# First expert layer in six units of two chunks and four of three, with seven short items to an attention slot, on one Trainium2 core

## What is computed

```python
for t in range(S):                      # 768 steps, 4 x 8 heads of 48
    S_re, S_im = ar*S_re - ai*S_im + k[t] (x) v[t],  ar*S_im + ai*S_re
    y[t] = q[t] @ S_re                  # a = (ar, ai), its magnitude clipped at 0.999
x = y as 3072 tokens x 384
h = x @ w_in                            # 384 -> 2048
x = (h * clip(h + 3, 0, 6) / 6) @ w_out # first layer
h = x @ w2_in
out = (max(h, 0) + alpha * min(h, 0)) @ w2_out   # second layer
```

## Time and profile before

| what | value |
|---|---|
| median of 3 runs | 1022.65 us (1019.16 to 1023.57) |
| the profiled execution's own time | 1022.65 us |
| its span, first to last instruction | 1020.9 us |
| busy: PE, PEld | 964.2 us, 864.4 us |
| busy: DVE, ACT, POOL | 598.6, 481.7, 265.5 us |
| mean granted TensorE clock | 0.986 of full speed |

### The profile page before, as it was taken

How to read it: one execution, slowest core, us unless ns; L and a number is a source line. 1 busy time by engine, 2 the same in 40 slices (tenths; PEclk the granted TensorE clock), 3 DMA queues, 4 the chain that set the end, 5 groups by cost and what they waited for, 6 DMA issues and landing times.

```text
span 1020.9 us, 17091 instructions
## 1 busy us (share of the span) xinstructions
PE 964.2 (94%) x6498; PEld 864.4 (85%) x6498; DVE 598.6 (59%) x1088; ACT 481.7 (47%) x865; POOL 265.5 (26%) x235
## 2 busy tenths in 40 slices
PE   0789988999999999999999999999999999999997
PEld 0678888889999999999999998888888888888886
DVE  6858888788787878878772245443433433434332
ACT  7746777666677667677742453221221222212211
POOL 0000122222222222322222333333333333323332
PEclk9789999999999999999999999999999999999999
DMA  6762323334333333432321701000010010100000
GB/s 168 204 148 71 87 71 83 94 86 118 76 94 84 76 94 96 97 94 71 82 68 24 272 31 55 0 31 33 1 63 1 1 62 1 62 1 1 32 1 31
DMA packets 80931, 70.49 MB, mean 69 GB/s; under 512 B 32592, under 2 KB 78160, under 8 KB 80464
## 3 DMA queue, kind: packets, MB, share of 16 engines
q1 hardware_dynamic: 77648, 66.42, 23.9%
q10 hardware_dynamic: 3200, 2.97, 1.2%
HBM read 40.90 MB, written 9.44 MB: 49 GB/s over the span
## 4 chain that ended last, share of the span: by engine, by line
PE 74%; DVE 10%; SPq 5%; ACT 4%; issue 3%; DMA 2%; DVEq 0%; ACTq 0%
PE op L1202 11%; PE op L1203 10%; PE hp L1203 10%; PE op L1204 10%; PE hp L1202 10%; PE hp L1204 10%; PE yp L1190 3%; SPq L413 2%; PE gp L1197 2%; DMA st<-prod 2%; PE op L1250 2%; PE gp L1169 2%; DVE t_fb L820 2%; SPq L416 1%; PE hp L1225 1%
## 5 line engine op out<-in xcount | busy, mean ns | idle before, releaser
L535 POOL TENSOR_TENSOR g_lo<-gated,g_hi 128x384 fp32r<-128x384 f32 (+2 forms) x224 | 263.3, 1176 | 746.0 <-ACT g_hi L631 746.0
L631 ACT ACTIVATE g_hi<-gated 128x384 fp32r<-128x384 f32 (+2 forms) x224 | 123.0, 549 | 327.2 <-DVE gated L918 284.4
L914 DVE TENSOR_SCALAR gate<-hp,alpha_sb 128x512 f32<-128x512 f32 x96 | 72.1, 751 | 239.9 <-PE hp L1204 239.9
L903 DVE SCALAR_TENSOR_TENSOR gated<-gate,hp 128x384 f32<-128x384 f32 (+1 forms) x144 | 72.9, 506 | 130.8 <-ACT gate L624 130.7
L1202 PE MATMUL op<-g_hi,wb_hi 128*128 128x384 f32 (+1 forms) x384 | 129.4, 337 | 2.9 <-POOL g_lo L535 2.6
L1202 PE MATMUL hp<-x_hi,wa_hi 128*128 128x384 f32 (+1 forms) x384 | 127.1, 331 | 3.8 <-DVE gated L903 2.9
L1204 PE MATMUL op<-g_hi,wb_lo 128*128 128x384 f32 (+1 forms) x384 | 124.5, 324 | 0.0
L1203 PE MATMUL op<-g_lo,wb_hi 128*128 128x384 f32 (+1 forms) x384 | 124.3, 324 | 0.0
L1203 PE MATMUL hp<-x_lo,wa_hi 128*128 128x384 f32 (+1 forms) x384 | 123.8, 322 | 0.0
L1204 PE MATMUL hp<-x_hi,wa_lo 128*128 128x384 f32 (+1 forms) x384 | 123.8, 322 | 0.0
L624 ACT ACTIVATE gate<-hp,half 128x384 f32<-128x384 f32 (+1 forms) x144 | 76.8, 533 | 95.7 <-PE hp L1204 81.0
(11 more groups left out here) (110 smaller groups left out, 1652.1 us busy)
## 6 DMA issues: line engine op xcount, KB each, us to landing
st<-prod SPq DMA_DIRECT2D x76, 145.1 KB, 3.0
a_sb<-a_in SPq DMA_DIRECT2D x24, 288.0 KB, 3.9
qk_sb<-qk_in SPq DMA_DIRECT2D x24, 288.0 KB, 3.6
v_pad<-v_in SPq DMA_DIRECT2D x24, 192.0 KB, 4.1
x_raw<-x SPq DMA_DIRECT2D x6, 768.0 KB, 5.6
out<-out_sb SPq DMA_DIRECT2D x6, 768.0 KB, 4.0
st<-prod SPq DMA_DIRECT2D x96, 32.2 KB, 2.3
wa_raw<-w_in SPq DMA_DIRECT2D x6, 512.0 KB, 6.4
```

The lines of the kernel that those rows point to most:

```text
L535: pool.tensor_tensor(g_lo[:, at, 0:wide], gated[:, at * UT:at * UT + wide], g_hi[:, at, 0:wide].bitcast(F32), ALU.subtract).then_inc(glo_d ...
L631: act.activation(g_hi[:, at, 0:wide], gated[:, at * UT:at * UT + wide], ACT.Copy).then_inc(ghi_done, 1)
L903: dve.scalar_tensor_tensor(out=gated[:, to], in0=gate[:, at], scalar=1.0, in1=hp[:, n % 2, 0:wide], op0=ALU.min, op1=ALU.mult).then_inc(ga ...
L914: dve.tensor_scalar(gate[:, at], hp[:, n % 2, 0:wide], 0.0, alpha_sb[:, m:m + 1], ALU.min, ALU.mult).then_inc(gate_done, 1)
```

## The change

The first layer has ten units in place of nine: six of two chunks and four of three, where three of two and six of three stood. It has 160 items in place of 144. Three items in place of two come ahead of the first slot, whose length goes from 7 to 6. Slots 3 to 10 have 7 items, slots 11 to 14 have 8, 7, 7 and 8, all of units of two chunks; before, slots 3 and 4 had 7, slots 5 to 8 had 6 (two-chunk units) and slots 9 to 14 had 5, 5, 6, 5, 5, 6 (three-chunk units). In long slots `forward` of a chunk moves from the end of the slot before to the first item of its own, and `squares` moves one item later (letter "s").

```diff
-SIZES = (2, 2, 2, 3, 3, 3, 3, 3, 3)
+SIZES = 6 * (2,) + 4 * (3,)
...
-SHORT = {6: ("a", "cf", "deo", "glv", "hij", "kb"), 7: ("a", "cf", "deo", "glv", "hi", "j", "kb")}
-LONG = {5: ("a", "cdefg", "ov", "hij", "klb"), 6: ("a", "cdefg", "ov", "hij", "klb", "")}
...
-ALONE = 2
-LENGTHS = (7, 7, 7, 6, 6, 6, 6) + 4 * (5, 5, 6) + (5, 6, 6)
+SHORT = {6: ("a", "cf", "deos", "glv", "hij", "kb"), 7: ("a", "cf", "deos", "glv", "hi", "j", "kb"),
+         8: ("a", "cf", "deos", "glv", "hi", "j", "kb", "")}
+LONG = {5: ("aB", "cdefg", "ov", "hijs", "kl"), 6: ("aB", "cdefg", "ov", "hijs", "kl", "")}
...
+ALONE = 3
+LENGTHS = (6,) + 8 * (7,) + (8, 7, 7, 8) + 2 * (5, 5, 6) + (5, 6, 6)
...
+            if s > FIRST and is_short(s - 1):
+                steps = steps.replace("B", "")
...
-                if "o" in steps and c3 is not None:
+                if "s" in steps and c3 is not None:
                     squares(c3)
...
-            gate1(3)
+            for n in range(1, ALONE):
+                gate1(n + GSTEP)
...
                     fractions(c1)
+                    if "B" in steps:
+                        forward(c1)
```

## The result

The changed kernel took 1019.13 us (median of 20 runs, 1014.28 to 1023.22) against 1022.68 us (20 runs) for the kernel before: a ratio of 0.9966, 95% interval [0.9953, 0.9979]. It is faster by 3.5 us where 9.6 were forecast, and 0.13 us above the range. The profiled execution took 1018.77 us, span 1017.1 us.

The account below looks back on a forecast made before the run. PE was taken as nearly always busy after the first third, with losses to win before slot 15. Terms -4.3 (start of slot 3), -0.8 (slots 4 to 8), -4.5 (slots 9 to 14) took 1022.65 to 1013.0 us; range 1008.5 to 1019.0.

Parts of the forecast that it names:

- the term 21.5 us for slot 6: Slot 6 with seven items for six: PE needs 20.6 us, 21.5 taken, a little over the need.
- the store of unit 1: On SP ahead of slot 6's restack: one item earlier than before, so it lets go sooner; no separate size given.
- The attention chain holds the short slots: Rival, slots 6 to 14: engines set the length, 22.6 us per seven-item slot; 1024.2 us, half of it 1018.6; chance 0.15.
- slots 9 to 14: Six slots now of two-chunk items: 130.6 us together against 135.1 before, a term of -4.5 us.
- slot 4: Seven items and seven weight splits in both orders: keeps its 23.56 us.
- slot 5: A seventh item fits into the 2.38 us wait at its end; DVE limits it, 25.3 us.
- slot 8: Seven items for six: PE needs 21.2 us, 21.5 taken.
- the price of a two-chunk item: PE's time per item of a two-chunk unit: 2.16 us, against 3.12 us for a three-chunk one.
- Items of one price at any width: Rival: weight loads bound PE, so 16 more items cost 3.12 us each; 1059.1 us, chance 0.01.
- the step with DVE and ACT in all short slots: Slower rival: seven-item slots run at slot 4's 23.56 us; 1031.6 us, chance 0.05.
- three items ahead: Before slot 2: extra item cuts PE's wait from 3.88 to 1.3 us, restores the clock; slot 3 starts 4.3 us earlier.
- letters "B" and "s": Moved `forward` and `squares` in long slots: taken at nothing; rival of a loss at unit borders, 1017.0 us, chance 0.04.

Follow-up runs that it names:

- leave_first: Changed kernel with ACT's copy of unit 1's sums moved ahead of the other steps of its item; 1013.43 us, ratio 0.9932.
- third_item: Changed kernel with slot 5 at six items and slot 6 at eight, so unit 1 ends in slot 6's third item; 1016.04 us, ratio 0.9945.
- old_letters: Changed kernel with `forward` and `squares` of the long slots back where they stood before; 1020.57 us, ratio 0.9987.
- dose_three: leave_first with three table loads (3.84 us of ACT work) ahead of the early copy of unit 1's sums; 1018.48 us, ratio 0.9977.
- alone_three: Kernel before with only three items ahead of slot 2 and six in it; 1019.44 us, ratio 0.9985.

## Why the prediction was wrong

- **The step that failed: slots 6 to 8, the term 21.5 us for slot 6.** Measured were 27.96, and 23.07 with the copy early. The prediction looked at what stands beside slot 6 on SP ("the store of unit 1 ... behind the second item now and not the third, so it lets go sooner") and missed that the same move puts ACT's copy behind `logs`, 3.4 us behind its gate, with `output(32)` waiting for it on PE. leave_first and third_item, two edits that share only this, take PE's wait away. leave_first comes to 1013.43 us where 1013.0 had been forecast; part of that nearness is luck, since its own kernel before was faster as well, and it gained 8.3 of the 9.6 us.
- **What it cost, in the profile.** PE's need in slot 6 is 20.6; 0.68 and 2.39 of waits make 23.7; the other 4.3 us are the low clock, 10.2 us long (with 3.4 us of it, in old_letters, 1.8). Against leave_first slot 6 is 4.9 us longer and slot 7 22.49 - 21.14 = 1.35. That is 6.2 us in these two executions, where the medians give 4.8 to 5.7 and the ratios 3.5: the changed kernel's profile has the longest low clock seen behind this wait.
- **The other half of slot 6's term** was small: without the late copy it took 23.07, because the chain and not PE ends it. "The attention chain holds the short slots" was right for this one and wrong for slots 8 to 14, in which PE is busy for over 99% of the time.
- **Right: slots 9 to 14** (130.79 for 130.6), slot 4 (23.56 for 23.56), slot 5 (25.14 for 25.3), slot 8 (21.13 for 21.5), the price of a two-chunk item (slot 9 with seven of them took 21.39 us, with PEld busy for 20.76 of it). Items of one price at any width are out; so is the step with DVE and ACT in all short slots.
- **Right in its place and off in its size: three items ahead.** The wait fell from 3.88 to 0.64 us, further than to 1.3, and the clock in slot 2 is 1.00. Slot 3 begins 5.9 us earlier where 4.3 were taken; of the 1.1 us kept back for DVE, 0.7 show one slot later (slot 3 took 24.65 us where 23.93 were taken). In medians it is 2.3 to 2.8: the sum took the wait of 3.88 us from one profile, and other executions of the same order have 2.34 and 0.65. So this term of the sum was 1.5 to 2 us too large for a median, next to the late copy the second part of the miss.
- **Off: letters "B" and "s".** Taken at nothing, they gain 1.0 us in the changed kernel; half of it makes good what the rest of the change adds there, and slot 15 to the end took 656.1 us where 656.7 were expected.
- The range took in a chain that holds every short slot, but no single late step with the clock behind it, and so ended 0.13 us short.

## What to carry to other kernels

When a table of lengths shifts which item of a slot closes a unit, go through every step tied to that item, on every engine, and read what now stands ahead of it in the same item: here a copy of 0.8 us that moved behind 3.4 us of other work, `logs` above all, cost 3.5 to 5.7 us. Put what frees a buffer for the bound engine first in its item. Look at a wait of some 2 us on TensorE not only for its length but for the clock around it, which here made 2.4 us into 4.2 (old_letters) or 6.7 (the changed kernel). And take the size of a wait from more than one execution before it goes into a sum: the one ahead of slot 2 was 3.88, 2.34 and 0.65 us in three profiles of one order.

## What was not expected of the hardware

The low clock behind a wait of nearly one length differs between executions: 3.4 us behind the 2.40 us wait of old_letters, 6.8 behind the 2.91 of dose_three, 10.2 behind the 2.39 of the changed kernel. Waits of 1.42 and 1.62 us had none behind them. Over all fourteen profiles, from slot 2 to slot 15, PE had 28 waits of 1.80 us or more, 27 of them with a low clock inside or behind them (the other is 2.36 us ahead of slot 6 of alone_three), and there was no other low clock in that stretch. The changed kernel's 20 runs spread over 9 us, those of the kernel before over 5.5.
